# Banded attention, a gated convolution and an MLP on one core: weight loads in pieces, half-width first tiles, and softmax inverse sums turned through a scratch in HBM

## What is computed

```python
scores = q @ k.T / 8 - slope[h] * dist          # outside the mask: -1e9
a = exp(scores - max);  a = a / (sum(a) + 1e-9)
x = (a @ v)                                     # [B, S, 512]
val = x @ w_val;  gate = sigmoid(conv5(x))      # causal, 5 taps
x = (gate * val) @ w_out
h = relu(x @ w_in);  gate = sigmoid(conv3(h))   # w_in: 512 x 1024
out = (h * gate) @ w_out2
```

## Time and profile before

| | |
|---|---|
| median of 3 runs | 295.96 us (295.88 to 296.44) |
| the profiled execution | 295.67 us, span 293.9 us |
| PE busy | 277.0 us, 94% of the span |
| VectorE, ScalarE busy | 183.4 us (62%), 160.8 us (55%) |
| GpSimd busy | 56.3 us (19%) |
| DMA | 22.37 MB |

### The profile page before, as it was taken

One profiled execution on the slowest core, in us unless ns is written; L12 is line 12 of the kernel. 1 busy time (PEld: TensorE's weight loads), 2 busy tenths in 40 slices (PEclk: granted clock), 3 DMA queues, 4 the chain that ended last, 5 costly groups with the idle time before them and its releaser, 6 DMA issues.

```text
span 293.9 us, 4615 instructions
## 1 busy us (share of the span) xinstructions
PE 277.0 (94%) x1600; PEld 210.1 (71%) x1600; DVE 183.4 (62%) x445; ACT 160.8 (55%) x362; POOL 56.3 (19%) x76
## 2 busy tenths in 40 slices
PE   0799999999999999999999999999999998999994
PEld 0344457777787777788888888877888886887783
DVE  1832267777999999126943396977700579998300
ACT  1051168888999988183354433759113568834401
POOL 1035001667832533033061000000000000000000
PEclk9999999999999999999999999999999999999998
DMA  6999312555554200000000000000003000000311
GB/s 221 404 334 334 138 37 51 182 165 156 183 167 145 76 2 2 0 7 0 0 0 2 0 0 2 1 0 0 0 2 143 0 0 3 0 0 0 143 73 71
DMA packets 11689, 22.37 MB, mean 76 GB/s; under 512 B 1680, under 2 KB 1680, under 8 KB 11408
## 3 DMA queue, kind: packets, MB, share of 16 engines
q1 hardware_dynamic: 11376, 22.03, 22.4%
q10 hardware_dynamic: 288, 0.02, 0.1%
HBM read 18.90 MB, written 3.15 MB: 75 GB/s over the span
## 4 chain that ended last, share of the span: by engine, by line
PE 68%; DVE 9%; issue 9%; POOL 7%; DMA 3%; ACT 2%; SPq 0%; POOLq 0%
PE ps L489 16%; PE ps L491 16%; PE ps L490 16%; PE ps L406 10%; DVE hgB L1020 4%; POOL w2l L350 4%; PE ps L452 3%; PE ps L424 3%; PE ps L435 3%; DMA win<-in_win 3%; DVE hgB L1027 2%; POOL w2h L348 2%; PE ps L461 1%; DVE hglA L1033 1%; POOL kW L335 1%
## 5 line engine op out<-in xcount | busy, mean ns | idle before, releaser
L621 ACT ACTIVATE prob<-prob,low 128x256 f32<-128x256 f32 x96 | 47.4, 501 | 1.7 <-DVE low L852 1.7
L1020 DVE SCALAR_TENSOR_TENSOR hgA<-h,cw,hgA 128x512 f32<-128x512 f32 x32 | 21.9, 747 | 26.5 <-ACT hgA L737 26.5
L406 PE MATMUL ps<-win,w1t 128*128 128x512 f32 x64 | 29.5, 621 | 9.3 <-DMA win<-in_win 9.3
L491 PE MATMUL ps<-gh,Wl 128*128 128x512 f32 x96 | 38.3, 399 | 0.0
L490 PE MATMUL ps<-gl,Wh 128*128 128x512 f32 x96 | 37.9, 394 | 0.0
L489 PE MATMUL ps<-gh,Wh 128*128 128x512 f32 x96 | 37.7, 392 | 0.0
L725 ACT ACTIVATE h<-ps 128x512 f32<-128x512 f32 x24 | 14.3, 597 | 40.7 <-PE ps L491 40.5
L876 DVE SCALAR_TENSOR_TENSOR g<-xT,cw,g 128x512 f32<-128x512 f32 x48 | 33.8, 755 | 1.7 <-ACT g L660 1.6
L852 DVE CUSTOM_DVE_ANT_0 prob<-ps,bias 128x256 f32<-128x256 f32 x80 | 29.1, 419 | 6.3 <-PE ps L424 6.2
L406 PEld LDWEIGHTS ps<-win,w1t 128*128 128x128 f32 x64 | 12.6, 201 | 24.9 <-issue 15.5
L424 PE MATMUL ps<-kW,q_rows 64*128 64x256 f32 x192 | 27.2, 402 | 0.0
(11 more groups left out here) (89 smaller groups left out, 521.9 us busy)
## 6 DMA issues: line engine op xcount, KB each, us to landing
q_rows<-in_q SPq DMA_DIRECT2D x12, 256.0 KB, 4.6
kW<-in_k SPq DMA_DIRECT2D x12, 256.0 KB, 4.6
v_own<-in_v SPq DMA_DIRECT2D x12, 256.0 KB, 2.9
out<-xT SPq DMA_DIRECT2D x6, 512.0 KB, 2.9
v_win<-in_v SPq DMA_DIRECT2D x12, 192.0 KB, 3.0
win<-in_win SPq DMA_DIRECT2D x2, 1024.0 KB, 9.5
w<-in_w SPq DMA_DIRECT2D x8, 256.0 KB, 11.1
w1t<-in_w1t SPq DMA_DIRECT2D x1, 1024.0 KB, 5.4
```

What stands on the lines that cost most here:

```text
L406: last = pe.matmul(WB(i), w1t[:, m, k * P:(k + 1) * P], win[:, m, half * 512:(half + 1) * 512], start=(m == 0), stop=(m == CT - 1))
L491: return pe.matmul(out, w_lo, x_hi, start=False, stop=final)
L621: act.activation(prob[:, f, i, :], prob[:, f, i, :], ACT.Exp, scale=-1.0, bias=low[:, f, i:i + 1], accum_out=total[:, t % 2, HH * f + i:HH ...
L1020: dve.scalar_tensor_tensor(out=raw, in0=h_cols(m, c, tap - 1), scalar=cw2[:, m, tap:tap + 1], in1=raw, op0=ALU.mult, op1=ALU.add).then_inc ...
```

## The change

1. **Loads.** w1t and the first half of win come in four pairs of pieces of 256 KB, each pair with its own semaphore, and PE does the first four products by pieces: it begins with the first pair. nw is issued by ACT. `WB(i)` is bank i, so that eight banks hold the eight products and the waits between them are gone. Six products stand ahead of `qk(0)` (seven before), and two among `qk(0)`, `qk(1)` and `transposes(0)`.
2. **First tiles.** Tiles 0 and 6 (the first of each batch) have no tile before them. Their window half is left out in `qk`, `scores`, `exps`, `transposes`, the copies and `pv`; its keys and values are not loaded for v_win.
3. **Inverse sums.** `widen`, `spread_inverse` and `copy_inverse` go. SP's `turn_inverse(t)` waits for `inverse(t)`, writes the 128 x 8 numbers to `inv_rows` in HBM with their order turned, waits until this is done, and loads the rows back, repeated over 64 partitions, with two transfers.
4. **PO** has two banks, `inv` and `invT` two slots, and `scale_x(t)` moves from round 2t+4 to round 2t+5.
5. **Convolution steps** start in round 13 and are two in odd rounds, one in even ones, one in the last.

```diff
-TAPS_FROM = 2 * (CHUNK_TILES[0] + 1)
+TAPS_FROM = 2 * (CHUNK_TILES[0] + 2)
-CONV_STEPS = {n: 2 if n % 3 == 0 and n < 2 * TILES - 5 else 1 for n in range(TAPS_FROM + 1, 2 * TILES)}
+CONV_STEPS = {n: 2 if n % 2 and n < 2 * TILES - 1 else 1 for n in range(TAPS_FROM + 1, 2 * TILES)}
...
-        PO = ps[:, 6, :].rearrange("p (j q) -> p j q", j=PAIRS)
-        IV = ps[:, 7, :].rearrange("p (j q) -> p j q", j=PAIRS)
-        WB = lambda i: ps[:, 2 + i % 4, :]
+        PO = lambda t: ps[:, 6 + t % 2, :].rearrange("p (j q) -> p j q", j=PAIRS)
+        WB = lambda i: ps[:, i, :]
...
-            sp.dma_start(nw[:, :], A_n.partition_broadcast(P)).then_inc(n_in, 16)
-            sp.dma_start(w1t[:, :, :], A_w1t).then_inc(w1_in, 16)
-            sp.dma_start(win[:, :, 0:F // 2], A_win[:, :, 0:F // 2]).then_inc(w1_in, 16)
-
+            for m in range(CT):
+                sp.dma_start(w1t[:, m, :], A_w1t[:, m, :]).then_inc(w1_in[m], 16)
+                sp.dma_start(win[:, m, 0:F // 2], A_win[:, m, 0:F // 2]).then_inc(w1_in[m], 16)
...
+            def turn_inverse(t):
+                slot = t % 2
+                sp.wait_ge(inverse_done, t + 1)
+                sp.dma_start(inv_rows[t].rearrange("h q -> q h"), inv[:, slot, :],
+                             allow_slow_non_contiguous=True).then_inc(inv_sent[slot], 16)
+                sp.wait_ge(inv_sent[slot], 16 * (t // 2 + 1))
+                if t >= 2:
+                    sp.wait_ge(x_ready, t - 1)
+                for e in range(2):
+                    sp.dma_start(invT[e * D:(e + 1) * D, slot, :, :], inv_rows[t, e:H:2, :].partition_broadcast(D)).then_inc(invT_in[slot], 16)
...
-            def widen(t):
-                pool.wait_ge(inverse_done, t + 1)
-                if t >= 1:
-                    pool.wait_ge(spread_done, t)
-                pool.tensor_copy(inv_wide[:, :, :], inv[:, :].unsqueeze(2).to_broadcast([P, H, D])).then_inc(wide_done, 1)
...
+            for m in range(CT):
+                pe.wait_ge(w1_in[m], 32)
+                for k in range(CT):
+                    last = part_W(k, m)
+                    if m == CT - 1:
+                        last.then_inc(w_mm, 1)
+            pe.wait_ge(win_in, 16)
+            product_W(CT)
+            product_W(CT + 1)
...
-            def spread_inverse(t):
-                pe.wait_ge(wide_done, t + 1)
-                if t >= 1:
-                    pe.wait_ge(invT_copied, t)
-                for j in range(PAIRS):
-                    last = pe.transpose(IV[:, j, :], inv_wide[:, 2 * j:2 * j + 2, :].rearrange("p e d -> p (e d)"), ident[:, :])
-                last.then_inc(spread_done, 1)
...
                 dve.wait_ge(pv_done, 2 * t + 2)
-                dve.wait_ge(invT_copied, t + 1)
-                dve.tensor_tensor(xT[:, :, t // TPB, x_at(t):x_at(t) + P], PO, invT[:, :, :], ALU.mult).then_inc(x_ready, 1)
+                dve.wait_ge(invT_in[t % 2], 32 * (t // 2 + 1))
+                dve.tensor_tensor(xT[:, :, t // TPB, x_at(t):x_at(t) + P], PO(t), invT[:, t % 2, :, :], ALU.mult).then_inc(x_ready, 1)
...
-                for n in range(1, HALF_TILES):
-                    if n % 2 == 0 and n >= 4:
-                        scale_x((n - 4) // 2)
+                for n in range(2, HALF_TILES):
+                    if n % 2 and n >= 5:
+                        scale_x((n - 5) // 2)
                     scores(n)
```

More of the change, by code:

```diff
@@ L165, in program @@
         OB = lambda c, m: ps[:, (0 if c == CHUNKS - 1 else 4) + m, :]
-        n_in, w1_in, win_in, wv_in, cw_in = sem("n_in"), sem("w1_in"), sem("win_in"), sem("wv_in"), sem("cw_in")
+        n_in, win_in, wv_in, cw_in = sem("n_in"), sem("win_in"), sem("wv_in"), sem("cw_in")
+        w1_in = [sem(f"w1_in{m}") for m in range(CT)]
         w2_in = [sem(f"w2_in{k}") for k in range(FT)]
@@ L285, in _ @@
                     load_w2(k)
[L286 to L289, removed]
+                for t in range(TILES):
+                    if t + RING < TILES:
+                        load_q(t + RING)
+                        load_k(t + RING)
+                    turn_inverse(t)
+                    if t + RING < TILES:
+                        load_v(t + RING)
             with sp.Else():
@@ L396, in _, with part_W @@
         def _(pe):
-            pe.wait_ge(w1_in, 32)
+            def part_W(i, m):
+                half, k = i // CT, i % CT
+                return pe.matmul(WB(i), w1t[:, m, k * P:(k + 1) * P], win[:, m, half * 512:(half + 1) * 512],
+                                 start=(m == 0), stop=(m == CT - 1))
             def product_W(i):
[L400 to L404, removed]
                 for m in range(CT):
-                    last = pe.matmul(WB(i), w1t[:, m, k * P:(k + 1) * P], win[:, m, half * 512:(half + 1) * 512],
-                                     start=(m == 0), stop=(m == CT - 1))
+                    last = part_W(i, m)
                 last.then_inc(w_mm, 1)
-            for i in range(2 * CT - 1):
-                product_W(i)
+            for m in range(CT):
[7 more added lines that the diff above has]
+            product_W(CT + 1)
             def qk(n):
@@ L423, in qk @@
                     pair, rows = 2 * f + i // 2, slice(i % 2 * D, i % 2 * D + D)
-                    last = pe.matmul(SC(f, i % 2)[:, i // 2, :], q_rows[rows, slot, pair, :], kW[rows, slot, :, pair, :],
+                    keys = kW[rows, slot, 1, pair, :] if first_of_batch(t) else kW[rows, slot, :, pair, :]
+                    last = pe.matmul(SC(f, i % 2)[:, i // 2, P if first_of_batch(t) else 0:KEYS], q_rows[rows, slot, pair, :], keys,
                                      start=True, stop=True)
@@ L433, in transposes @@
                     for i in range(2):
-                        for c in range(2):
+                        for c in key_parts(n // 2):
                             last = pe.transpose(PT(j)[:, (2 * i + c) * P:(2 * i + c + 1) * P],
@@ L520, in _ @@
                     qk(n)
[L521 to L522 removed]
                     transposes(n - 1)
+                    if n == 2:
+                        pe.wait_ge(wl_done, 2 * CT)
                     pv(n - 2)
@@ L612, in _ @@
                 act.activation(wvh[:, k, :], wval[:, k, :], ACT.Copy).then_inc(wvh_done, 1)
-            for i in range(2, 2 * CT - 1):
+            for i in range(CT + 2):
                 copy_W(i)
@@ L973, in _ @@
                 scores(0)
-                split_W(2 * CT - 1)
+                split_W(CT + 2)
+                scores(1)
+                split_W(CT + 3)
+                copy_t1(0)
                 next_step = 0
-                for n in range(1, HALF_TILES):
-                    if n % 2 == 0 and n >= 4:
-                        scale_x((n - 4) // 2)
+                for n in range(2, HALF_TILES):
+                    if n % 2 and n >= 5:
+                        scale_x((n - 5) // 2)
                     scores(n)
```

106 lines of the change are left out of this document (55 added, 51 removed).

## The result

The changed kernel takes **366.1 us** (median of 4 runs, 363.39 to 369.08) against 296.2 us (295.88 to 297.46) before: a ratio of 1.232, with a 95% interval of 1.224 to 1.240. The profiled execution took 366.09 us, its span 364.2. The result is 70 us slower, where 12.7 us less were forecast, and 54 us more than even the slow rival gave.

What follows compares the result with a forecast made beforehand. PE was taken to bound the kernel, with VectorE close behind and setting the pace in later rounds. First val_part at 104.4 instead of 116.56 gains 12.2 us, the last spread 0.5: 12.7 less, 283.3 us, range 280.3 to 291.

Steps and rivals of the forecast that it cites:

- the slow rival: Attention rounds: at 93 ns a piece the turn of 11.6 to 12 us sets the pace; about 312 us, chance 0.1.
- I take the small packets' 16 ns: Write of the inverse sums: 16 ns for each extra piece, 0.9 us added to 2.9, so 3.8 us to landing.
- its upper bound, 93 ns for each small piece: Write of the inverse sums: each piece priced like a 2 KB packet, making the whole turn 11.6 us.
- The rule of the Trainium skill that was set aside: Turned write: one descriptor per element, far slower than the hardware's transpose; forecast said it would cost nothing, turn 7.1 us.
- Every us above that costs half a us for each tile, since two tiles are in flight: Attention rounds: cost of each us by which the turn, forecast at 7.3 us, exceeds its slack of 7.9 to 8.1.
- SP reaches the write in time, as it waits before it only for `qk(2t+2)`: SP's stream in the rounds: that wait is over before inverse(t), so no delay to the write was counted.
- the first rival: Attention rounds: turn somewhat longer than its slack, 8 to 10.4 us; 287 us at 9, 292 at 10; chance 0.2.
- Behind the rounds: After the first val_part: x all there at +9.7 us, a turn of up to 10 us hides, last spread saves 0.5.
- The spread that is gone: Behind the first val_part on PE: the last spread of the inverse sums goes, 0.5 us gained.
- its slack: Attention rounds: time from the end of inverse to scale_x, 8.1 us in VectorE's rounds, 7.9 in PE's, hiding the turn.

Runs made afterwards that it cites:

- experiment 5: Changed kernel with the inverse sums written as 256 pieces of 16 bytes, issued by ScalarE, and invT read with a stride: 293.49 us, ratio 0.990.
- experiment 2: Changed kernel with the turn of the inverse sums, the PO bank and the place of scale_x as before, other parts kept: 289.01 us, ratio 0.975.
- experiment 9: Changed kernel with each inverse sum stored twice, so the turned write has 1024 pieces of 8 bytes, issued by SP: 323.85 us (one run).
- experiment 3: Changed kernel with the inverse sums written by SP as 128 pieces of 32 bytes, unturned, so x is scaled wrongly: 294.01 us (one run).
- experiment 4: Changed kernel with the write of the inverse sums issued by ScalarE instead of SP: 350.75 us (one run).
- experiment 7: Kernel before with added transfers behind attention: piece spacings of 8 to 64 bytes, 16-byte pieces, a load behind the turned write; load landed after 11.7 us, alone 2.7.
- experiment 1: Kernel before with small transfers added behind attention on SP, each waited for: 296.75 us; the turned write of 1024 pieces landed after 9.3 us.

## Why the prediction was wrong

**Where it held.** PE starts at 5.22 us (4.8 was forecast), `qk(2)` at 36.62 (36.4), `qk(4)` at 41.73 (41.4). A half-wide `qk` takes 0.65 us in the chain (0.7). That `qk(2)` came within 0.2 us is in part luck: `qk(0)` was 0.8 late (27.71 against 26.9), and the stretch behind it took 8.9 us in place of 9.5. Rounds of 3.11 us are there in experiment 5, the pace of 6.94 us from round 15 in experiment 2. Each of these had a row of the same work behind it.

**The first step that failed: "I take the small packets' 16 ns".** The write was priced at 3.8 us, and its upper bound, 93 ns for each small piece, at 8.1 us. It took 10.0 in the kernel (median; 8.5 to 10.9) and 9.3 alone. The error was not in the size of a packet's time: that is 12 ns at most, near what was taken. It was to take the landing of a write as its packets' time plus a constant. Neither the queue rows nor any bound made from them could hold the 5.6 us or more that come behind the last packet, and the price hangs on how close the pieces lie (9.3 us at 4 bytes, 4.3 at 8, 2.5 at 64), which no row had. The rule of the Trainium skill that was set aside, against turning data by a rearranged access pattern, was the right warning; its measured time per packet, 7.1 us for the whole turn by the estimate, was not: the last turn, which waits for nothing else, takes 15.5 us from the issue of the write at 181.89 to the data at 197.35.

**The second: "Every us above that costs half a us for each tile, since two tiles are in flight".** Two slots of `inv` and `invT` exist, but one stream serves them. SP waits for write t, then issues its read and five loads, and only then write t+1. So there is one write in flight, and the period is the time from its issue to its landing plus 3.8 us of issues: on average over the first eight, 13.7 us in the profile, 10.2 in experiment 9, 7.3 in experiment 3. With the predicted write it would have been some 3.8 + 3.8 = 7.6 (an estimate), above VectorE's 6.94: even at the predicted price this wait would have set the pace. The slow rival has the same flaw. With the measured 15.5 us its sum gives 39 + 5 x 21 = 144 for `inverse(10)` and a first `val_part` near 149; it came at 180.04.

**The third: "SP reaches the write in time, as it waits before it only for `qk(2t+2)`".** The list of SP's waits left out the one that the change adds, for its own write. The inverse sums of 98.84 wait until 108.45 for SP. The wait that the change adds to SP's stream also holds what is queued behind it: the read, five loads and the next write.

**The fourth: what a slow write does to its neighbours.** The sum has no term for it; only the first rival says that the loads share the queue. The loads of k in the changed kernel land after 6.2 us and those of v after 4.8; for v it was 2.9. Experiments 4 and 7 show the cause at its plainest. How much this adds in the changed kernel was not measured by itself; the chain there goes through the writes and SP's issues, not through the loads.

**Behind the rounds** a turn of up to 10 us should hide. The last write is issued at 181.89, 1.85 us after the first `val_part`, and the end of the chain reads:

```profile
193.35 3.91 DMA invT<-inv_rows
197.35 0.70 DVE xT L888
198.08 0.64 ACT xh L670
198.79 1.28 POOL xl L377
200.20 0.76 PE ps L511
```

x is all there 16.2 us after the issue of the write, and PE waits for it:

```profile
200.20 0.76 PE L511 MATMUL ps<-xh,wvh 128*128 128x512 f32 x1 [2.86 <-POOL xl L377]
```

But this wait is only 2.9 of the 6.8 us. The first `val_part` and the transposes behind it take 6.6 us (180.04 to 186.61), where they took 3.8 before (116.56 to 120.40): PE had been idle for 5.3 us ahead of them, and the granted clock is 0.55 here and was 1.00 there. In the same way the first seven matmuls behind the wait take 3.0 us (to 203.21) in place of 1.7. The spread that is gone gives 0.5 back. The step was right in its form and failed with the price, and with it came a lower clock that it had not counted.

**The sum of the loss.** 63.5 us in the rounds and 6.8 behind them are the 70.3 us by which the span grew (364.2 - 293.9). Against it stand the 7.3 us that the other parts gain by themselves. Part of the 63.5 is the lower clock of a PE that idles; it is not a loss of its own, since PE is not in the chain there.

**Open.** Whether 283 us can be had with a turn through HBM. In experiment 5 write and reads are short and the first `val_part` still comes at 115.32, not 104.4, 10.9 us later. Three parts of this are on record: `qk(2)` is 0.9 late, VectorE's four waits for invT sum to 6.3, and ten longer `scale_x` (0.39 each) add 3.9 at most. They would cover it, but no run separates them, and only where VectorE sets the pace does a longer `scale_x` count in full. The turn there is still longer than its slack for some tiles, since the read is issued 2.0 to 5.2 us behind the write. More turns in flight, and gaps of 4 bytes between the sums within the kernel, weren't tried.

## What to carry to other kernels

Price a small transfer by the landing of one with the same pieces, at the same distance from each other, not by packet times: single floats turned in HBM landed after 9 to 11 us, the same 4 KB in pieces of 16 or 32 bytes after 1.4 to 3.2 by themselves and about 3 at the median within a kernel. When a stream issues a transfer and then waits for it, add up one whole turn of that stream, issues included, and hold it against the pace of the engines; slots in memory don't overlap what one stream does in single file. And when a change has several parts, time them apart: here the other parts gained 7 us, and the turn hid them under a loss of 77.

## What the runs showed of the hardware

- A write of 1024 single floats to HBM, one transfer at a time, lands after 8.8 and 9.7 us with neighbours 4 bytes apart (experiment 1; 10.8 with a load right behind it, experiment 7), 4.3 at 8, 3.0 at 16, 2.8 at 32, 2.5 (turned) to 3.4 (in order) at 64, and 2.9 into on-chip memory. Half the pieces, turned, take as long (9.1). In the first of these writes 5.6 of the 8.8 us pass with no packet on record.
- Such a write delays the transfers behind it, from its own issuer (11.7 in place of 2.7 us, experiment 7) and from another (in experiment 4 loads land after 10.6 and 10.9 us, in the changed kernel after 4.8 and 6.2).
- The same 4 KB in pieces of 32 bytes land in 1.4 us, in pieces of 16 bytes in 1.5 and 3.2 (two each).
- VectorE's product with a float operand at a stride of 16 bytes takes 1082 ns for 128x512 (experiment 5), and 692 with it in a row; at a stride of 8 bytes it takes 691 (experiment 9).
